# Attention steps by table and moved rests in a fused attention and two-layer feed-forward kernel

## The reference

```python
def _attn_ref(q, k, v, g_norm):                    # 4 x 8 x 576 x 64
   kv = np.einsum('bhsd,bhse->bhde', k, v)
   out = np.einsum('bhsd,bhde->bhse', q, kv)
   rms = np.sqrt(np.mean(out * out, axis=-1, keepdims=True) + 1e-06)
   return (out / rms * g_norm).astype(np.float32)

def _moe_ref(x, w_in, w_out):                      # 2304 x 512, d_ff 2048
   h = x @ w_in
   g = h * (1.0 / (1.0 + np.exp(-h)))
   return (g @ w_out).astype(np.float32)

def _moe2_ref(x, w_a, w_b, w_out):                 # d_ff 1536
   return ((x @ w_a) * (x @ w_b) @ w_out).astype(np.float32)
```

## Time and profile before

| | |
|---|---|
| median of 3 runs | 893.97 us (893.73 to 895.67) |
| the profiled execution | 895.0 us, its span 893.2 us |
| instructions | 17059 |
| busy in the span | TensorE 98%, VectorE 57%, ScalarE 31%, GpSimd 69% |
| mean granted clock of TensorE | 0.998 |

### The profile page before, as it was taken

How to read it: one execution, slowest core, us unless ns; L and a number is a source line. 1 busy time by engine, 2 the same in 40 slices (tenths; PEclk the granted TensorE clock), 3 DMA queues, 4 the chain that set the end, 5 groups by cost and what they waited for, 6 DMA issues and landing times.

```text
span 893.2 us, 17059 instructions
## 1 busy us (share of the span) xinstructions
PE 872.3 (98%) x6626; PEld 824.4 (92%) x6626; DVE 512.3 (57%) x813; ACT 279.9 (31%) x467; POOL 618.0 (69%) x901
## 2 busy tenths in 40 slices
PE   7999999999999999999999999999999999999998
PEld 6799889998999999999989899999988999999996
DVE  2767556647786666655765355454473554545536
ACT  2864344534443323222431221121151211211210
POOL 1666545555487777776688697897889876877760
PEclk9999999999999999999999999999999999999999
DMA  9760505111111111111101021011110250111103
GB/s 269 183 146 25 128 25 104 49 48 34 40 38 36 47 48 48 49 48 48 48 25 48 24 61 59 24 49 50 45 48 25 94 131 24 54 49 40 48 26 106
DMA packets 47103, 55.63 MB, mean 62 GB/s; under 512 B 11952, under 2 KB 32432, under 8 KB 47024
## 3 DMA queue, kind: packets, MB, share of 16 engines
q1 hardware_dynamic: 44304, 49.55, 20.1%
q10 hardware_dynamic: 2720, 4.98, 1.9%
HBM read 49.81 MB, written 4.72 MB: 61 GB/s over the span
## 4 chain that ended last, share of the span: by engine, by line
PE 89%; DVE 4%; POOL 2%; issue 2%; DMA 1%; ACT 1%; SPq 1%; DVEq 0%; ACTq 0%; POOLq 0%
PE ps L733 44%; PE ps L803 8%; PE ps L805 7%; PE ps L804 7%; PE ps L825 5%; PE ps L827 5%; PE ps L826 5%; PE ps L750 3%; PE ps L690 2%; DMA kvq<-in_q_dram 1%; PE ps L700 1%; PE ps L664 1%; POOL w_lo L481 1%; PE ps L678 1%; DVE ps L1354 0%
## 5 line engine op out<-in xcount | busy, mean ns | idle before, releaser
L733 PE MATMUL ps<-x_hi,w_hi 128*128 128x288 f32 x1064 | 230.5, 298 | 5.0 <-ACT kept L1062 2.3
L733 PE MATMUL ps<-x_lo,w_hi 128*128 128x288 f32 x1064 | 228.7, 297 | 0.0
L733 PE MATMUL ps<-x_hi,w_lo 128*128 128x288 f32 x1064 | 227.4, 295 | 0.0
L733 PEld LDWEIGHTS ps<-x_hi,w_hi 128*128 128x128 f32 x1064 | 175.2, 189 | 17.2 <-issue 5.0
L733 PEld LDWEIGHTS ps<-x_hi,w_lo 128*128 128x128 f32 x1064 | 172.2, 189 | 0.0
L733 PEld LDWEIGHTS ps<-x_lo,w_hi 128*128 128x128 f32 x1064 | 171.0, 189 | 0.0
L479 POOL TENSOR_SCALAR w_hi<-wt 128x256 fp32r<-128x256 f32 x152 | 69.4, 457 | 129.9 <-PE ps L733 123.6
L803 PE MATMUL ps<-g_hi,d_hi 128*128 128x288 f32 x512 | 155.1, 303 | 2.9 <-ACT qT_sb L1002 1.1
L1390 DVE TENSOR_TENSOR xy<-xy,ps 128x288 f32<-128x288 f32 x224 | 100.8, 453 | 93.2 <-PE ps L805 92.2
L1062 ACT COPY kept<-ps 128x576 f32<-128x576 f32 x114 | 73.2, 642 | 253.0 <-PE ps L733 252.2
L805 PE MATMUL ps<-g_hi,d_lo 128*128 128x288 f32 x512 | 150.8, 295 | 0.0
(11 more groups left out here) (102 smaller groups left out, 1230.4 us busy)
## 6 DMA issues: line engine op xcount, KB each, us to landing
raw<-in_moe_w_out_dram SPq DMA_DIRECT2D x28, 512.0 KB, 3.8
raw<-in_moe_w_in_dram SPq DMA_DIRECT2D x15, 512.0 KB, 3.6
raw<-in_moe_w_a_dram SPq DMA_DIRECT2D x12, 512.0 KB, 3.6
raw<-in_moe_w_b_dram SPq DMA_DIRECT2D x12, 512.0 KB, 3.6
kvq<-in_k_dram SPq DMA_DIRECT2D x12, 288.0 KB, 5.0
kvq<-in_v_dram SPq DMA_DIRECT2D x12, 288.0 KB, 6.0
out_dram<-xy SPq DMA_DIRECT2D x27, 128.0 KB, 2.4
kvq<-in_q_dram SPq DMA_DIRECT2D x16, 144.0 KB, 6.0
```

The source lines that it names most:

```text
L733: mm = pe.matmul(ps[:, bank + s, 0:PART], w, x[:, n, c, s * PART:(s + 1) * PART], start=(begins and first), stop=last, skip_group_check=no ...
```

## The change

The steps of each unit of the second group's attention come from tables now (`KV_AT`, `Q_AT`, `PROD_AT`, `ROOT_AT`, `RESULT_AT`), and banks are counted for each unit (`unit_turn`) in the order in which TensorE meets units and tiles. The kv of heads 1 to 3 moves from steps 12, 24 and 36 to 8, 17 and 27, and the other units of these heads with it; at steps 10 and 11 two units stand in one step. The root of a head from head 1 on stands on ScalarE behind the third `part` of a pair (steps 16, 30 and 44). The loads of head 2 go behind weight load 5 instead of 6. VectorE's `second_pair` gets one `attend`. At the three changes of segment the rest of x for n = 3 goes from GpSimd to VectorE; in layer 1 the rests for n = 2 and 3 stand behind `silu(pp, 3)`, in layer 2 the rest for n = 3 is VectorE's last step. At the change from pair 15 to 16, `g_round(15, 3)` and `g_rest(15, 3)` move into pair 16, behind ScalarE's first `part` and VectorE's first flush.

```diff
@@ -57,8 +57,12 @@
-    SLOTS = 12
-    SLOT_BANKS = (2, 1, 1, 1, 1, 1, 1, 0, 0, 1, 1, 1)
+    KV_AT = (0, 8, 17, 27)
+    Q_AT = ((1, 2, 3), (10, 11, 12), (21, 22, 23), (28, 29, 31))
+    PROD_AT = ((4, 5, 6), (13, 14, 15), (24, 25, 26), (35, 36, 37))
+    ROOT_AT = (7, 16, 30, 44)
+    RESULT_AT = ((9, 10, 11), (18, 19, 20), (32, 33, 34), (46, 47, 48))
@@ -77,9 +81,9 @@
     FIRST_ROUNDS = ((0, 0), (7, 0), (0, 1), (7, 1), (3, 0), (6, 0), (3, 1), (6, 1), (5,), (1,), (2,), (4,))
-    POOL_RESTS = (((0, 0), (0, 1), (7, 0), (7, 1), (5, 0), (5, 1)), (3, 6))
+    POOL_RESTS = (((0, 0), (0, 1), (7, 0), (7, 1), (5, 0), (5, 1)), (6,))
     DVE_RESTS = (((3, 0), (6, 0), (3, 1), (6, 1), (1, 0), (1, 1), (2, 0), (2, 1), (4, 0), (4, 1)),
-                 (0, 1, 2, 4, 5))
+                 (0, 1, 2, 3, 4, 5))
@@ -307,15 +311,23 @@
-        slot_turn, tile_turn, turns = [], [], 0
+        def units(at, steps):
+            return [(h, j) for h in range(PAIRS) for j in range(JS) if steps[h][j] == at]
+        unit_turn, tile_turn, turns = {}, [], 0
         for pp in range(PAIR0[-1] + 1):
...
             for n in range(steps):
-                slot_turn.append(turns)
-                at = STEPS * pp + n
-                turns += SLOT_BANKS[at % SLOTS] if n < STEPS and at < SLOTS * PAIRS else 0
+                if n < STEPS:
+                    at = STEPS * pp + n
+                    turns += 2 * KV_AT.count(at)
+                    for kind in (RESULT_AT, Q_AT, PROD_AT):
+                        for unit in units(at, kind):
+                            unit_turn[kind, unit] = turns
+                            turns += 1
                 for _ in range(0 if pp == 0 else PLAIN_TILES_AFTER if pp == 1 else TILES_AFTER[n]):
@@ -326,8 +338,8 @@
-        def slot_bank(at):
-            return BANK_D + slot_turn[at] % 2
+        def unit_bank(kind, h, j):
+            return BANK_D + unit_turn[kind, (h, j)] % 2
@@ -446,7 +458,7 @@
                     load_heads(1)
-                if r == 6:
+                if r == 5:
                     load_heads(2)
@@ -501,8 +513,6 @@
                 ready(u, 2, t0)
-                if u == PROD0[seg_of(pair_of(u))]:
-                    x_rest(seg_of(pair_of(u)), 3)
                 ready(u, 3, b21)
@@ -703,17 +713,14 @@
-                h, a = divmod(at, SLOTS)
-                if h >= PAIRS:
-                    return
-                if a == 0:
-                    kv(1, h)
-                elif a <= 3:
-                    q_turn(1, h, a - 1, slot_bank(at))
-                elif a <= 6:
-                    q_kv(1, h, a - 4, slot_bank(at))
-                elif a >= 9:
-                    o_turn(1, h, a - 9, slot_bank(at))
+                if at in KV_AT:
+                    kv(1, KV_AT.index(at))
+                for h, j in units(at, RESULT_AT):
+                    o_turn(1, h, j, unit_bank(RESULT_AT, h, j))
+                for h, j in units(at, Q_AT):
+                    q_turn(1, h, j, unit_bank(Q_AT, h, j))
+                for h, j in units(at, PROD_AT):
+                    q_kv(1, h, j, unit_bank(PROD_AT, h, j))
@@ -1001,23 +1008,21 @@
-            def attend(at, evict):
-                h, a = divmod(at, SLOTS)
-                if at >= STEPS * PAIR0[1] or h >= PAIRS:
-                    return
-                if not evict:
-                    if a == 7:
-                        root(1, h)
-                elif a == 0:
-                    kv_keep(1, h)
-                elif a <= 3:
-                    qT_keep(1, h, a - 1, slot_bank(at))
-                elif a <= 6:
-                    square(1, h, a - 4, slot_bank(at))
-                    o_keep(1, h, a - 4, slot_bank(at))
-                elif a >= 9:
-                    keep(1, h, a - 9, slot_bank(at))
+            def attend(at):
+                if at in KV_AT:
+                    kv_keep(1, KV_AT.index(at))
+                for h, j in units(at, RESULT_AT):
+                    keep(1, h, j, unit_bank(RESULT_AT, h, j))
+                for h, j in units(at, Q_AT):
+                    qT_keep(1, h, j, unit_bank(Q_AT, h, j))
+                for h, j in units(at, PROD_AT):
+                    square(1, h, j, unit_bank(PROD_AT, h, j))
+                    o_keep(1, h, j, unit_bank(PROD_AT, h, j))
+            def second_root(at):
+                if at in ROOT_AT:
+                    root(1, ROOT_AT.index(at))
@@ -1095,38 +1100,39 @@
...
             def second_pair():
                 at = STEPS
-                attend(at, False)
+                second_root(at)
+                attend(at + 1)
                 sigmoid(1, 0)
-                attend(at + 2, True)
+                attend(at + 2)
                 first_round(5)
                 g_round(1, 0)
-                attend(at + 3, True)
+                attend(at + 3)
                 first_round(1)
                 sigmoid(1, 1)
-                attend(at + 4, True)
+                attend(at + 4)
                 g_round(1, 1)
                 first_round(2)
-                attend(at + 5, True)
+                attend(at + 5)
                 sigmoid(1, 3)
-                attend(at + 6, True)
+                attend(at + 6)
                 g_round(1, 3)
                 sigmoid(1, 2)
                 g_round(1, 2)
@@ -1134,45 +1140,39 @@
                 u, at = prods_of(pp)[0], STEPS * pp
-                attend(at, True)
+                attend(at)
                 part(u, 0)
...
                     g_round(pp - 1, 3)
-                attend(at, False)
                 next_round(pp, 0)
-                attend(at + 1, True)
+                attend(at + 1)
                 part(u, 1)
-                attend(at + 1, False)
                 next_round(pp, 1)
-                attend(at + 2, True)
+                attend(at + 2)
                 part(u, 2)
-                attend(at + 2, False)
+                second_root(at + 2)
                 last_round(pp)
                 next_round(pp, 2)
-                attend(at + 3, True)
-                attend(at + 3, False)
+                attend(at + 3)
                 sigmoid(pp, 0)
-                attend(at + 4, True)
+                attend(at + 4)
                 next_round(pp, 3)
                 g_round(pp, 0)
-                attend(at + 4, False)
                 sigmoid(pp, 1)
                 g_round(pp, 1)
-                attend(at + 5, True)
+                attend(at + 5)
                 next_round(pp, 4)
-                attend(at + 5, False)
                 sigmoid(pp, 2)
-                attend(at + 6, True)
+                attend(at + 6)
                 next_round(pp, 5)
                 g_round(pp, 2)
-                attend(at + 6, False)
                 sigmoid(pp, 3)
-                if SEGS[seg_of(pp + 1)][1] == 2:
-                    g_round(pp, 3)
...
                 part(ua, 0)
+                if pp == PAIR0[2]:
+                    g_round(pp - 1, 3)
                 part(ua, 1)
@@ -1269,19 +1269,16 @@
             def attend(at):
-                h, a = divmod(at, SLOTS)
-                if at >= STEPS * PAIR0[1] or h >= PAIRS:
-                    return
-                if 4 <= a <= 6:
-                    sums(1, h, a - 4)
+                for h, j in units(at, PROD_AT):
+                    sums(1, h, j)
...
-                h, a = divmod(at, SLOTS)
-                if at < STEPS * PAIR0[1] and h < PAIRS and 8 <= a <= 10:
-                    if a == 8:
-                        invert(1, h)
-                    normalise(1, h, a - 8)
+                for h, root_at in enumerate(ROOT_AT):
+                    if 1 <= at - root_at <= JS:
+                        if at - root_at == 1:
+                            invert(1, h)
+                        normalise(1, h, at - root_at - 1)
@@ -1337,7 +1334,7 @@
                 if pp == PAIR0[seg]:
-                    x_rest(seg, DVE_RESTS[1][3 + n])
+                    x_rest(seg, DVE_RESTS[1][4 + n])
@@ -1504,13 +1502,12 @@
                 attend(at + 6)
-                next_rest(pp, 2)
                 add(u, 2, both(BANK_C))
...
                 silu(pp, 3)
-                if SEGS[seg_of(pp + 1)][1] == 2:
-                    g_rest(pp, 3)
+                next_rest(pp, 2)
+                next_rest(pp, 3)
                 if pp in (5, 6):
@@ -1522,6 +1519,7 @@
                 flush(0, 0)
+                g_rest(pp - 1, 3)
                 late_rest(pp, 0)
```

More of the change, by code:

```diff
@@ L1097, in first_pair @@
                 half_round(6, 1)
-                attend(0, True)
+                attend(0)
                 sigmoid(0, 0)
-                attend(1, True)
+                attend(1)
                 g_round(0, 0)
                 sigmoid(0, 3)
-                attend(2, True)
+                attend(2)
                 g_round(0, 3)
                 sigmoid(0, 1)
-                attend(3, True)
+                attend(3)
                 g_round(0, 1)
-                attend(4, True)
+                attend(4)
```

(17 more changed lines are left out.)

## The result

The changed kernel takes 886.97 us in the median (886.03 to 888.83), the kernel before 893.97: a ratio of 0.9924 (95% interval 0.9906 to 0.9942). The forecast was 886.6 us, 882.5 to 890.4, so the time came out as forecast. Its parts did not: the attention gave more than its term, the segment changes gave less, and the two errors cancelled: that the total came so close is luck. The profiled execution took 886.97 us, span 885.1.

The account below looks back on a forecast made before the run. TensorE, busy 872.3 of 893.2 us, was taken as the bound, so only its waits and slow clock could be won. Terms -4.85 + 1.3 + 0 - 3.8 = -7.35 took 893.97 to 886.6 us, range 882.5 to 890.4.

Parts of the forecast that it names:

- the attention: Second group's attention, 80 to 235 us: banks, root and two worse places in sum -4.85 us.
- the segment changes: Rests moved from GpSimd to VectorE at three pair changes: +1.3, 0 and -3.8 us.
- Banks: Steps 18 to 47: 13 tile waits on the wrong bank go, 4.3 us, less 0.4 for units at a sixth step.
- Root: Head 1's root, moved from step 19 to 16: table loads no longer delay the transposes, 1.7 us gone.
- Steps 14 and 46: Pair 2's first step and pair 6: longer waits on a ScalarE copy and a first normalisation, +0.35 and +0.4 us.
- Loads: Loads of heads: third ahead of a weight load, fourth landing at 135.4 us, needed near 141.5; no cost.
- rival D: First product of the fourth head waits for its load, landing near 151: 896 us or more; chance 0.03.
- Pair 21 to 22: Rest moved to VectorE: TensorE's 2.06 us split wait and 1.7 us of low clock go, -3.8 us.
- Pair 7 to 8: Rest moved to VectorE: third and fifth tiles wait for flushes, with restarts 1.7 us; net +1.3.
- rival B: Rests collide, VectorE bounds: one clock fall at pair 16 (1.7), 0.9 more waits, 889.2 us; 0.18, plus 0.04 near 893.6.
- Pair 15 to 16: Rest moved to VectorE, rounding moved: 2.3 us of old waits go, 2.3 of flush waits come, sum 0.
- Rival A: VectorE keeps up at both changes, pairs 8 and 16; no tile waits for a flush: 882.6 us; chance 0.15.

Follow-up runs that it names:

- the bank counts alone: The kernel before, with only the bank count read from each unit's own step: 889.22 us, ratio 0.9943.
- the attention alone: The changed kernel with every move at the three segment changes undone: 888.98 us, ratio 0.9931.
- the flushes first: The changed kernel with flushes of the new pair's first tiles ahead of moved rests, g_rest and late rest at pairs 8 and 16: 883.87 us, ratio 0.9880.
- the changed kernel's second profile: The changed kernel unaltered, run once more beside the kernel before on the same chip: 888.47 us, ratio 0.9919.

## Why the prediction was right, and where it was not

**Banks: right, too small.** Forecast -4.3 with 0.4 back, measured -5.1 by the ratio and -5.3 start by start. The thirteen tile waits were counted and priced well; the slower product behind was priced well too (0.07), but it stood at 17 tiles. And the 0.4 for units at the sixth step of a pair never came: no start is late at steps 19, 33 and 47. That term was argued from ScalarE's order without asking when the bank is wanted next, which is a tile later: at step 19 of the changed kernel the copy is over at 113.74 us, and the second tile starts at 113.96.

**Root: right.** -1.7 forecast; when the tables alone were taken away, 1.64 went in the trace and 2.0 by the ratio.

**Steps 14 and 46: right in sign, and for 46 by the wrong cause.** Forecast +0.35 and +0.4, measured +0.17 and +0.16 to 0.3. The tile of step 14 is 1.04 late, the transposes of step 46 0.89, where some 1.2 and 1.1 were forecast. At step 46 I blamed the reciprocal and the first normalisation; the run that moved the half sum showed that it was a flush behind them, the one that the list of waits names.

**Loads: right.** The heads land in at most 6.0 us in the changed kernel's trace, and no wait for them stands in its list from 80 to 235 us; rival D is out.

**Pair 21 to 22: the wait right, the clock mis-sized.** Of -3.8, the wait of 2.06 us went whole. The 1.7 of slow clock was put down to the wait because the fall stood right behind it in the one trace that I had the earlier trace rows. In the profiles with the bank counts alone and with the attention alone, the same wait of 2.0 us has no fall behind it. Of 63 executions of kernels with that wait 18 have a mean clock of 0.999 or 1.0, 30 of about 0.998, 15 of 0.996 or less; of 39 without it, 25, 14 and none. One fall is 0.002. So the wait makes a fall behind it more frequent and not certain, and another one comes early in the kernel whatever stands at pair 22. Where the fall does stand behind the wait it cost 1.3 to 1.7 us start by start (the kernel before beside the one with the bank counts alone), so its price was right, and it was wrong to count it in each execution. In the median the clock gives back some 1.0 to 1.4 us: the 0.6 to 1.1 that the segment changes gain by the ratios, and the 0.35 that they lose in waits.

**Pair 7 to 8: right mechanism, 0.6 too small.** Forecast: 1.7 of waits and restarts, less 0.4. Measured: starts late by 1.00 and 1.34, less the same 0.4. This term was mis-sized. The first was forecast as 0.4; the two rests in front of it took 1.56 and 1.89 us where the sum had 1.6 and 1.35, which is 0.5 of it. The spread of a rest was in the bounds (up to 3.7 us), and the value I took was too low for rests that run beside weight splits (with the flushes first, the second of them starts behind the split and takes 1.34). The Trainium skill, page "SBUF — State Buffer", section "Who interferes with whom", calls the port pair that VectorE and GpSimd share an exclusive lock, by which one engine would wait for the other's whole instruction. The rest of 1.89 us against 1.35 agrees as to the direction. Of rival B, at 889.2, one term nearly came, the 0.9 more of waits (0.6 here and 0.2 at pair 16); the other, a fall of the clock at pair 16, did not: the granted clock is 1.00 there.

**Pair 15 to 16: right.** 2.3 less 2.3 was forecast; 1.00 and 1.44 came for what was 0.6 and 1.67.

**The sum.** -6.2 for the attention (forecast -4.85) and -0.6 to -1.1 for the segment changes (forecast -2.5) make -6.8 to -7.3: the forecast's -7.35, by errors of about 1.4 to 1.9 against each other. What the two terms of the segment changes hide is seen start by start, from the kernel with the attention alone to the changed one, two profiles with no fall at either place: 2.05 us lost at pair 8 and 0.24 at pair 16, 1.94 won at pair 22. In waits the moves are worth nothing (0.35 lost). That their gain is falls of the clock that no longer come follows from the counts above; no run shows it by itself. Rival A, that no tile would wait for a flush, was wrong for this change, yet its time, 882.6, is about what the order with the flushes first and pair 8's late rest moved reached (882.4).

## What to carry to other kernels

When a step moves to another engine, write down what stands between the last free moment of that engine and each thing that a third engine waits for, and put the new step behind all of these, not only behind the first: here the same rests cost some 5 us in one order that they don't cost in another (ratios 0.9924 and 0.9866), and of two moves by one place one only handed the wait to the next instruction, and the other left it as it was. Take the releaser that the list of waits names, and ask what stands in front of that instruction on its engine; I had taken the instruction that I expected there. And a low clock behind a wait in one execution is not yet the price of that wait: count it over executions of kernels that have it and of kernels that don't.

## What the runs showed of the chip

TensorE's clock falls in some executions of a kernel and not in others, 3.4 us at a time, in these profiles at two places: behind the 2.0 us wait at pair 22 (starting 0.3 and 1.3 us after the wait's end in the two profiles that show it), and 19.6 to 20.8 us into the kernel, in the first group's attention (four profiles). The early one delays what follows by 0.95 to 1.3 us start by start. In the changed kernel's second profile TensorE was busy 1.59 of 3.60 us just before it (TensorE's busy time, clock, DMA share, GB/s):
```profile
16.00:19.60 3.60, 1.59 (x74) 1.00 1.05 346
```
That share alone does not tell: in the four profiles with an early fall it is 1.59 to 2.05 us of this stretch, in the eight without one 1.83 to 2.22. Three profiles of kernels with the wait show no fall behind it. What decides between executions no run here shows; it stays open.

GpSimd's rounding of a weight half, 0.41 us alone, takes 1.51 us where it meets a rest of VectorE, and the rest itself 1.79 where its shortest is 1.35; both stand in the changed kernel's trace at pair 22:
```profile
667.57 1.51 POOL L491 TENSOR_SCALAR w_hi<-wt 128x256 fp32r<-128x256 f32 x1
...
670.69 0.41 POOL L491 TENSOR_SCALAR w_hi<-wt 128x256 fp32r<-128x256 f32 x1
```
```profile
667.03 1.79 DVE L1324 TENSOR_TENSOR x_lo<-qT_sb,x_hi 128x1152 fp32r<-128x1152 f32 x1
```
TensorE waited for no split there: it is busy 15.97 of 16 us in that stretch.
